# Attention, experts and MLP in one kernel: the MLP's staged weight loads issued at other places of GpSimd's program

## What is computed

```python
attn_out = softmax(masked(q @ k.T / 8)) @ v        # 4 x 8 heads, 576 positions, local or strided mask
x = attn_out.transpose(0, 2, 1, 3).reshape(2304, 512)
# experts: 8 of them, D = 512, F = 1024
do_compute = x @ w_skip > 0                        # about half of the 2304 rows
e_idx, gate_w = argmax and softmax value of xc @ w_gate
out[do_compute] = xc + gate_w * (relu(xc @ w1[e_idx]) @ w2[e_idx])
# MLP on all rows: 512 -> 2048 -> 512
h = out @ w_in
return maximum(0.01 * h, h) @ w_out
```

## Time and profile before

| | us |
|---|---|
| median of 3 runs | 759.31 (758.33 to 766.53) |
| the profiled execution, its own time | 760.97 |
| span in its profile (one core, mean granted clock 0.977) | 759.2 |

### The profile page before, as it was taken

The page is one execution under the profiler, slowest core; times in us unless marked ns, Lnnn a source line. Parts: engine busy times, 40 slices in busy tenths (PEclk is TensorE's granted clock), DMA queues, the critical chain, the costliest instruction groups (busy, mean ns, idle before and its releaser), DMA issues.

```text
span 759.2 us, 12315 instructions
## 1 busy us (share of the span) xinstructions
PE 717.4 (94%) x4674; PEld 666.5 (88%) x4674; DVE 276.5 (36%) x597; ACT 231.7 (31%) x505; POOL 186.9 (25%) x173
## 2 busy tenths in 40 slices
PE   5999999785998999999999999999999999999997
PEld 4999989675998999998999999998989999998996
DVE  5767767458213111113233223323232332323222
ACT  2667665241111111122223222322232222223222
POOL 6231110104277776761200300110030011001000
PEclk9999999695999999999999999999999999999999
DMA  8484855573778989950100200110020001001001
GB/s 177 106 186 115 231 125 149 154 270 112 258 246 288 316 283 308 304 189 21 42 1 0 84 1 1 42 42 1 0 83 0 0 26 57 0 1 42 1 1 41
DMA packets 68648, 81.68 MB, mean 108 GB/s; under 512 B 26137, under 2 KB 47417, under 8 KB 68602
## 3 DMA queue, kind: packets, MB, share of 16 engines
q1 hardware_dynamic: 60040, 58.60, 26.0%
q0 software_dynamic: 7504, 22.44, 9.0%
q10 hardware_dynamic: 1058, 0.02, 0.1%
HBM read 68.84 MB, written 12.21 MB: 107 GB/s over the span
## 4 chain that ended last, share of the span: by engine, by line
PE 89%; ACT 2%; issue 2%; DVE 2%; DMA 2%; another core or an unknown queue 1%; POOL 0%; SPq 0%; ACTq 0%; POOLq 0%; DVEq 0%
PE psum L1680 26%; PE psum L1697 26%; PE psum L1565 10%; PE psum L1581 9%; PE psum L1443 4%; PE psum L1464 4%; ACT kt L884 2%; PE psum L1453 2%; PE psum L1415 1%; DMA q_st<-in_q_dram 1%; PE psum L1505 1%; PE psum L1522 1%; PE psum L1434 1%; PE psum L1598 1%; PE psum L1591 1%
## 5 line engine op out<-in xcount | busy, mean ns | idle before, releaser
L1380 DVE SCALAR_TENSOR_TENSOR g_act<-g_raw 128x384 f32<-128x384 f32 x96 | 53.6, 558 | 229.4 <-ACT g_raw L1019 229.4
L1680 PE MATMUL psum<-x2h,wih 128*128 128x384 f32 x384 | 130.7, 340 | 1.5 <-issue 1.5
L1680 PE MATMUL psum<-x2h,wil 128*128 128x384 f32 x384 | 129.4, 337 | 0.0
L1680 PE MATMUL psum<-x2l,wih 128*128 128x384 f32 x384 | 128.9, 336 | 0.0
L1019 ACT ACTIVATE g_raw<-psum 128x384 f32<-128x384 f32 x96 | 47.2, 492 | 235.7 <-PE psum L1680 235.7
L1697 PE MATMUL psum<-woh,g_l 128*128 128x512 f32 x288 | 114.0, 396 | 0.0
L1697 PE MATMUL psum<-wol,g_h 128*128 128x512 f32 x288 | 113.7, 395 | 0.0
L1697 PE MATMUL psum<-woh,g_h 128*128 128x512 f32 x288 | 112.2, 390 | 0.5 <-DVE g_l L1384 0.5
L857 POOL DMA_INDIRECT out_dram<-o_sb,idxo x15 | 16.0, 1066 | 282.7 <-ACT o_sb L1014 279.7
L1565 PE MATMUL psum<-xt,wring 128*128 128x160 f32 x512 | 82.4, 308 | 1.7 <-issue 1.7
L1581 PE MATMUL psum<-hp,wring 128*128 128x160 f32 x512 | 78.4, 299 | 1.1 <-ACT hp L974 0.6
(11 more groups left out here) (210 smaller groups left out, 875.6 us busy)
## 6 DMA issues: line engine op xcount, KB each, us to landing
wring<-in_moe_w_dram SPq DMA_DIRECT2D x64, 512.0 KB
x_sb<-x_rows SPq DMA_DIRECT2D x4, 1024.0 KB, 6.2
stage<-in_moe_w_in_dram POOLq DMA_DIRECT2D x4, 1024.0 KB, 6.4
stage<-in_moe_w_out_dram POOLq DMA_DIRECT2D x4, 1024.0 KB, 8.1
q_st<-in_q_dram SPq DMA_DIRECT2D x7, 576.0 KB
k_st<-in_k_dram SPq DMA_DIRECT2D x7, 576.0 KB
vs<-in_v_dram SPq DMA_DIRECT2D x20, 128.0 KB, 8.2
x_rows<-xo SPq DMA_DIRECT2D x8, 288.0 KB, 7.4
```

What stands on the lines that cost most here:

```text
L1380: dve.scalar_tensor_tensor(out=g_act[:, f % 2, :], in0=g_raw[:, f % 2, :], scalar=LEAK, in1=g_raw[:, f % 2, :], op0=ALU.mult, op1=ALU.max) ...
L1680: last = pe.matmul(bank[f % 2][:, 0:MT * P], wt[:, c, f * P:(f + 1) * P], xp[:, T.par, c, :], start=(c == 0 and n == 0), stop=(c == KD - 1 ...
```

## The change

The two first `stage_load`s are issued before the first gather, behind a wait for the last of the router's transposes of `x_sb`; every later load, `stage_load(i + 2)`, is issued directly behind `stage_split(i)`, after its subtraction has ended, where it was `stage_load(i + 1)` ahead of `stage_split(i)`.

```diff
@@ -730,10 +730,6 @@
-            pool.wait_ge(s_plan, 1)
-            carry()
-            gather_x(0, 0)
-
             def stage_load(i):
@@ -779,7 +775,12 @@
+            pool.wait_ge(s_rt, NT)
             stage_load(0)
+            stage_load(1)
+            pool.wait_ge(s_plan, 1)
+            carry()
+            gather_x(0, 0)
             for i in range(2 * NU):
@@ -802,13 +803,12 @@
-                if i + 1 < 2 * NU:
-                    if i:
-                        pool.wait_ge(s_stl, i)
-                    stage_load(i + 1)
                 if i == 0:
                     pool.wait_ge(s_tok_o, 2)
                 stage_split(i)
+                if i + 2 < 2 * NU:
+                    pool.wait_ge(s_stl, i + 1)
+                    stage_load(i + 2)
                 if i:
                     put_done(i - 1)
```

## The result

| | before | changed |
|---|---|---|
| median, 20 runs each | 760.3 us (758.13 to 766.53) | 764.89 us (760.12 to 769.71) |
| ratio | | 1.0054, 95% interval 1.0038 to 1.0070 |
| span of the profiled execution | 759.2 us | 763.3 us |

The kernel became slower by 0.54%, some 4 us. I had forecast 759.0 us with a range up to 763.3 us: the sign and the size are wrong, and the result lies above the range, though within the 1% to which I had given 0.93. Of the 5.9 us between 759.0 and 764.89, 1.0 us is the kernel before itself: its median of 20 runs is 760.3, and I had built on 759.31 from three. The rest is the 4.6 us between the two medians and the 0.3 us of gain that I had forecast.

A forecast was written before the change was run, and what follows sets the result against it. PE bounds the kernel, so the edit pays or costs only where PE waits for POOL. First gather -0.1, T2 +0.5, T3 -0.66 gave -0.3 us, so 759.31 became 759.0 us, range 755.7 to 763.3.

The forecast's parts named there:

- What bounds, and where it can pay: PE is 89% of the chain; only its waits for POOL can pay: 4.95 us in T2 to T5, plus the first gather.
- Part 1: Loads 0 and 1 before the first gather: gather not delayed, 0.1 us of gain, ends 0 and 0.5.
- Part 2: Later loads' issue moved to the iteration's end: fits POOL's idle time, added wait some 0.15 us, gain 0.66 us in T3.
- The gain in T3: Subtraction over at 248.9, so yr and the indirect DMAs come about 0.8 us sooner: gain 0.66 us, other end 0.
- Part 3: 1 MB ahead of each gather in the same queue: cost 0.5 us in T2, ends 0 and 4.3.
- my lower way: T2's gather is never seen before load 3 is down, so its second half comes 0.4 to 2.2 us late.
- B: Each gather waits for its load: 4.3 us in T2, 1.9 in T3, 0.5 in T4, 766.0 us; chance 0.16.
- Its upper end in T2: Load 3's landing of 8.6 us plus the gather's own full 3.7 us: 244.0 against 239.7, costing 4.3 us.
- A: In T2 to T5 the load's issue itself holds ACT's late relus; removing it gains 2.98 us, 756.3 us; chance 0.22.
- C: Two early issues hold up the router's tail at 162 to 164: +1.7 us, 761.0 us; chance 0.08.
- D: Loads were early enough at both places, only order changes: 759.3 us; chance 0.12.

The follow-up runs named there:

- e4_load2_mid: The changed kernel with load 2 back behind iteration 1's scatters and sort; 759.96 us, 1.0034 of the kernel before.
- the pair: One more profiled execution each of the kernel before and the changed kernel, unedited, on one chip; 756.0 us and 761.74 us.
- e3_load3_mid: The changed kernel with load 3 back behind T2's gather, scatters and sort; 759.95 us, 1.0028 of the kernel before.
- e2_late_only: The changed kernel with loads 0 and 1 back in their old places, only loads 2 to 7 moved; 761.55 us, 1.0052 of the kernel before.
- g2: The changed kernel with all sorting in iteration 0 and load 3 halved, 512 KB ahead of T2's gather and 512 KB behind; 0.9986 of before.
- f2_load_behind_gather: The changed kernel with load 2 behind iteration 1's sort and loads 3 to 7 directly behind their iteration's gather; 757.36 us, 1.0000 of before.
- f4_sort_in_T0_change: The changed kernel with all 18 indirect DMAs of the sort in iteration 0; 757.64 us, 0.9999 of the kernel before.
- e1_early_only: The changed kernel with loads 2 to 7 back in their old places, only loads 0 and 1 early; 757.6 us, 1.0007 of before.

## Why the prediction was wrong, point by point

**What bounds, and where it can pay.** Right: only the gathers touch PE. T2 was named as the tile with the largest loss.

**Part 1.** Right as far as it can be told: 1.0007 (0.9986 to 1.0028), and the first gather is undelayed. The 0.1 us of gain is too small for these runs.

**Part 2.** The load's 0.84 us fit into POOL's idle time, as foreseen. I priced the added wait at 0.15 us without a row for it; the rows show 0.30 us (L741 behind `wil`). And `yr` of T2 comes 0.8 us later in its tile (229.31 less 221.83 is 7.48, 230.23 less 221.95 is 8.28). Half of it is iteration 1 running later: its subtraction ends 7.85 us into T2 instead of 7.43, and with load 2 back in its old place (`e4_load2_mid`) 7.44. The other half is the signal held in `put_done`, 0.40 us. I had named `put_done` as standing behind that wait, and had not asked what another engine was waiting for there. The gain in T3 did not come. The gate copy there is short (0.17 us), but not for the reason that I gave: the subtraction ended at 249.44, not 248.9, and the copy came only at 251.95, because T2 had become 3.5 us longer. T3 did not get faster (19.99 against 19.52, and 18.86 in both profiles of the pair).

**Part 3, the step that failed.** I had the gather's second half landing at 240.1 to 241.9; PE turned it at 242.21. Then I took only 0.5 us of cost, because ACT's relu was late to 243.75 anyway and the gather could hide behind it. The cover is no property of the kernel: in the second profile of the kernel before, T3 to T5 take 18.86 us and T2 pays in full for its wait. The full delay counts, and it was longer than the 0.4 to 2.2 us of my lower way: 2.6 us in the pair. And no term of my sum held the clock. All rows of before that I read stood at 1.00 in the experts stage, and I did not ask what a longer wait does to it. In the pair it nearly doubled the price: 2.6 us of wait, 2.3 us of slower matmuls. So where the sum had 0.5 us for T2, T2 took 3.5 and 4.9 us more.

**The rivals.** *B* was nearest in time (766.0) and had the right cause, 1 MB ahead of the gather. Its upper end in T2, 4.3 us, lies between the 3.5 and 4.9 us measured, but by luck: it was all wait, and the wait grew by 2.6 us; the clock, which *B* did not have either, made up the rest. Its places in T3 and T4 did not come, since T2's stretching gives POOL its lead back; only where T2 is healed does T3 pay (`e3_load3_mid`). I should have given it more than 0.16. *A* is refuted: in T3 of the changed kernel a late relu ran 1.6 us after the last sort issue's end with no load near it, and T3 to T5 kept their losses.

```profile
262.04 0.97 POOL L756 DMA_INDIRECT sorted_rows<-rec,pos_i  x1 [0.30 <-issue]
264.58 0.30 ACT L974 ACTIVATE hp<-psum 128x160 f32<-128x160 f32 x1 [1.27 <-remote]
```

*C* is refuted by the profile: from the last transposes of x_sb to the first gather the router took 15.29 us before (161.01 to 176.30) and 15.25 changed (161.15 to 176.40). The timed interval of part 1 alone, up to 1.0028, would not exclude its 1.7 us. *D* holds for part 1 only.

In the second profile of the changed kernel load 3 landed at 237.9 us and the two halves of the gather behind it at 239.1 and 240.9. The Trainium skill's rule on order that I had weighed (page "DMA: Bandwidth & Descriptors", section "Queues, rings and completion order", where it stands for the queues of SP and ACT: a ring's descriptors are taken in order and an increment lands only behind the engine's earlier writes) agrees with that trace. It does not account for the halved load, which landed at 230.9 us, 5.3 us ahead of the gather that it stood before.

The gate copy that began 0.01 us behind the subtraction took 4.54 us, and in `e2_late_only` the one that began at 225.45, 0.02 us ahead of it, took 0.17 us. The Trainium skill's rule on the shared port pair (page "SBUF — State Buffer", section "Who interferes with whom": of a GpSimd instruction and a DVE copy in a two-port mode, whichever issues first has the pair to its end) agrees with these rows; in which mode the copy ran, no profile shows.

**Left open.** What made ACT's relus late in the first two profiles; how the loss divides between loads 2 and 3, which the timed intervals don't separate; the exact share of the held signal; whether the delay goes with the bytes ahead, which `g2` speaks against; and why the clock falls in one execution and not in another.

## What to carry to other kernels

A large load put at the earliest place where its buffer is free can end up directly ahead of a small transfer that another engine waits for; ask of each new place what is issued next on that queue, and put the load behind that instead (here that took the loss away, and won nothing over the kernel before). A new wait holds back cheap signals behind it as well as work. And price a wait of TensorE by what the clock does after it too, and never count on a delay seen in a single profile as cover.

## What the hardware showed that I had not expected

The length of PE's waits alone does not tell whether the clock falls behind them. Waits for the gather of 0.52 and 1.54 us left it at 1.00, and so did 1.10 and 1.15 us in `f2_load_behind_gather` and 1.87 us in `g2_sortT0_load3_halved`; waits of 3.11 and 1.13 us were followed by a stretch of 4 us at 0.50 and one at 0.73. In `f4_sort_in_T0_change`, with waits of only 1.56 and 0.22 us in the rows, it fell all the same:

```profile
236.00:240.00 4.00, 2.22 (x19) 1.82 (x18) 0.42 (x1) 0.46 (x2) 3.91 (x2) 1.00 1.02 343
240.00:244.00 4.00, 4.00 (x19) 4.00 (x19) 0.07 (x1) 0.30 (x1) 2.69 (x2) 0.57 0.62 204
```

So it did in `e1_early_only`, behind waits of 1.08 and 1.44 us with loads 2 to 7 where the kernel before has them:

```profile
244.00:248.00 4.00, 4.00 (x22) 4.00 (x21) 0.00 (x0) 0.00 (x0) 3.91 (x2) 0.68 0.69 249
```

In `f4_sort_in_T0_change` PE had been busy for 2.22 of the 4 us from 236 to 240; in the second profile of the kernel before it was busy 2.04 of the same 4 us, and the clock stayed. That executions of one and the same kernel fall on either side is likely from this, but no two profiles here show it.

The rest of the experts stage differed as well: T3 to T5 lost 0.66, 1.18 and 0.64 us in the first profile and nothing in the second profile of the same kernel.
